# Attention, slot mixture and squared-ReLU layer on one core: a place in SBUF freed early for one slice of mixing weights, half an expert in the tokens' place, expert weights in longer rows, and combine weights transposed elsewhere

## What is computed

```python
# 1. attention: batch 4, heads 8, 768 positions, head size 64
scores = q @ k.T / 8 - slope[h] * dist;  keep: first 8 keys, or 0 <= row - col < 96
x = softmax(scores) @ v                      # as 3072 tokens x 512
# 2. soft mixture: 8 experts with 4 slots each, F = 1024
logits = x @ phi                             # 3072 x 32
d = softmax over the tokens; slot_input = d.T @ x              # 32 x 512
slot_out[e] = relu(slot_input[e] @ w1[e]) @ w2[e]              # w1 512x1024, w2 1024x512
x = softmax over the slots (logits) @ slot_out
# 3. x = relu(x @ w_in) ** 2 @ w_out          # w_in 512x2048, w_out 2048x512
```

## Time and profile before

| | us |
|---|---|
| median of three runs | 513.3 (512.65 to 513.88) |
| the profiled execution, its own time | 512.37 |
| its span, first to last instruction | 510.6 |
| TensorE busy | 485.2 (95%) |
| VectorE busy | 363.6 (71%) |
| ScalarE busy | 346.4 (68%) |
| GpSimd busy | 95.1 (19%) |
| chain that ended last, TensorE's share | 80% |

### The profile page before, as it was taken

One profiled execution on the slowest core, in us unless ns is written; L12 is line 12 of the kernel. 1 busy time (PEld: TensorE's weight loads), 2 busy tenths in 40 slices (PEclk: granted clock), 3 DMA queues, 4 the chain that ended last, 5 costly groups with the idle time before them and its releaser, 6 DMA issues.

```text
span 510.6 us, 12851 instructions
## 1 busy us (share of the span) xinstructions
PE 485.2 (95%) x4608; PEld 399.3 (78%) x4608; DVE 363.6 (71%) x1026; ACT 346.4 (68%) x761; POOL 95.1 (19%) x223
## 2 busy tenths in 40 slices
PE   2999999999999998869989999999999999999997
PEld 1767766776766642325879999999999999999996
DVE  6687786786786662226998978777777877768783
ACT  2788887887888710004999887777677777777740
POOL 1555544554454404120000000000000000000000
PEclk9999999999999999999999999999999999999999
DMA  7699889884465599997001011010110101001011
GB/s 287 245 348 355 348 292 320 328 333 151 151 207 162 202 352 407 391 387 283 0 1 43 1 43 42 0 41 0 41 38 3 41 0 41 5 36 41 0 42 42
DMA packets 24587, 77.24 MB, mean 151 GB/s; under 512 B 2400, under 2 KB 2400, under 8 KB 22112
## 3 DMA queue, kind: packets, MB, share of 16 engines
q1 hardware_dynamic: 19536, 60.95, 32.8%
q10 hardware_dynamic: 5008, 15.73, 8.3%
HBM read 70.39 MB, written 6.29 MB: 150 GB/s over the span
## 4 chain that ended last, share of the span: by engine, by line
PE 80%; ACT 6%; DVE 3%; SPq 3%; DMA 3%; issue 2%; POOL 2%; ACTq 0%; DVEq 0%; POOLq 0%
PE bank L1579 14%; PE bank L1578 14%; PE bank L1580 14%; PE bank L1251 8%; PE bank L1239 5%; PE bank L1266 4%; PE bank L1550 4%; SPq L387 3%; PE bank L1271 3%; ACT probs L990 3%; PE bank L1301 2%; DMA w_b<-w_dram 2%; POOL probs L443 2%; PE bank L1234 2%; PE bank L1509 2%
## 5 line engine op out<-in xcount | busy, mean ns | idle before, releaser
L990 ACT ACTIVATE probs<-probs,nmax 128x232 f32<-128x232 f32 (+1 forms) x192 | 88.6, 462 | 33.6 <-DVE nmax L533 33.6
L443 POOL TENSOR_SCALAR probs<-probs,rden 128x232 f32<-128x232 f32 (+1 forms) x192 | 83.0, 453 | 92.0 <-DVE rden L542 92.0
L1578 PE MATMUL bank<-t_hi,s_hi 128*128 128x256 f32 x352 | 98.7, 280 | 0.0
L1579 PE MATMUL bank<-t_lo,s_hi 128*128 128x256 f32 x352 | 98.6, 280 | 0.0
L1580 PE MATMUL bank<-t_hi,s_lo 128*128 128x256 f32 x352 | 98.5, 280 | 0.0
L533 DVE CUSTOM_DVE_ANT_0 probs<-bank,bias 128x232 f32<-128x232 f32 (+1 forms) x192 | 61.7, 378 | 25.5 <-PE bank L1239 22.1
L1113 ACT ACTIVATE g_s<-bank 128x1024 f32<-128x1024 f32 x48 | 49.0, 1022 | 30.2 <-PE bank L1550 30.2
L1142 ACT ACTIVATE s_hi<-s 128x512 fp32r<-128x512 f32 x88 | 55.0, 627 | 18.5 <-DVE s L917 14.6
L1578 PEld LDWEIGHTS bank<-t_hi,s_hi 128*128 128x128 f32 x352 | 66.5, 189 | 0.0
L1579 PEld LDWEIGHTS bank<-t_lo,s_hi 128*128 128x128 f32 x352 | 66.4, 189 | 0.0
L1580 PEld LDWEIGHTS bank<-t_hi,s_lo 128*128 128x128 f32 x352 | 66.4, 189 | 0.0
(11 more groups left out here) (189 smaller groups left out, 995.3 us busy)
## 6 DMA issues: line engine op xcount, KB each, us to landing
qkv_s<-qkv_dram SPq DMA_DIRECT2D x15, 1028.0 KB, 7.6
qkv_s<-qkv_dram SPq DMA_DIRECT2D x16, 704.0 KB, 4.9
w_s<-w_dram ACTq DMA_DIRECT2D x5, 2048.0 KB, 11.4
w_s<-w_dram SPq DMA_DIRECT2D x15, 512.0 KB, 8.5
out_dram<-o_stage SPq DMA_DIRECT2D x24, 256.0 KB, 2.0
w_a<-w_dram SPq DMA_DIRECT2D x9, 512.0 KB, 10.3
wo_raw<-w_out_dram SPq DMA_DIRECT2D x4, 1024.0 KB, 13.6
w_pre<-w_dram ACTq DMA_DIRECT2D x1, 2048.0 KB, 10.1
```

The source lines that it names most:

```text
L443: last = pool.tensor_scalar(probs[:, v % 2, m, a, 0:w], probs[:, v % 2, m, a, 0:w], rden[:, v % 2, m, a:a + 1], 1.0, ALU.mult, ALU.mult)
L990: act.activation(probs[:, v % 2, m, a, 0:w], probs[:, v % 2, m, a, 0:w], ACT.Exp, bias=nmax[:, v % 2, m, a:a + 1], scale=-1.0, accum_out=d ...
L1578: pe.matmul(OUT[n], hi, W_HI[n](at_f), start=(c == 0 and f == 0 and n in (0, 2, 4, 5)), stop=False, skip_group_check=True)
L1579: pe.matmul(OUT[n], hi, W_LO[n](at_f), start=False, stop=False, skip_group_check=True)
```

## The change

- The bias tables are split in heads 0 to 5 and heads 6 and 7. The first six heads' tables are no longer read when three steps of the last batch are left; the second 1 MB slice of w_in (`win_a[1]`) goes there. SyncE issues it, and `win_c[1]`, ahead of blocks 4 and 5 of expert 2. The other slice, `win_a[0]`, stays where the 2 MB `win_a` was issued.
- The first half of w2 of expert 7 goes into the tokens' place in REG_C (`w2_c`), behind `slots_1`, the last reading of the tokens. The second half (`w2_b`) follows the last chunk of w1.
- w2 is laid out as `e (p c) n`: partition p holds rows 8 p to 8 p + 7, and a load of n blocks has rows of 2n KB. `ht_g` reads `h_s` with a step of 8 elements to match. w_out is laid out in pairs of rows (4 KB), and mix is written in that order, from PSUM with a step of 2 elements.
- `W2_PARTS` are 4, 2, 1 and 1 blocks, of three experts each (6 MB in all).
- `parts(0)` stands behind `l2_0`, `parts(1)` behind `l1_1`, `parts(2)` ahead of block 0 and `parts(3)` ahead of block 4 of `l2_1`. VectorE's `spread` (3 operations) moves from ahead of `relu_0` to behind the copy of `parts(2)`.

```diff
@@ REG_A, REG_B, REG_C
-        bias = at(REG_A, "bias", [P, HEADS, KW])
-        bias0 = at(REG_A, "bias0", [P, HEADS, P])
+        bias_last = at(REG_A, "bias_last", [P, 2, KW])
+        bias0_last = at(REG_A, "bias0_last", [P, 2, P])
+        win_1 = cursor[REG_A]
+        bias0_first = at(REG_A, "bias0_first", [P, HEADS - 2, P])
+        bias_first = at(REG_A, "bias_first", [P, HEADS - 2, KW])
...
+        win_at = win_1 - 8192
-        win_a = at(REG_A, "win_a", [P, DC // 2, FF])
+        win_a = [at(REG_A, "win_a0", [P, FF], start=win_at), at(REG_A, "win_a1", [P, FF])]
-        w2_b = at(REG_B, "w2_b", [P, FEC, D], start=0)
+        w2_b = at(REG_B, "w2_b", [P, FEC // 2, D], start=0)
+        w2_c = at(REG_C, "w2_c", [P, FEC // 2, D], start=8192)
-        W2_PARTS = ((0, 2), (2, 4), (4, 6), (6, 7), (7, 8))
+        W2_PARTS = ((0, 4), (4, 6), (6, 7), (7, 8))
-        w2_v = w2.rearrange("e (c p) n -> e p c n", p=P)
+        w2_v = w2.rearrange("e (p c) n -> e p c n", p=P)
@@ SyncE
             load_w2(2, 0, 4)
+            if windowed:
+                sp.wait_ge(biased, 8 + BATCH * (2 * UNITS) - 4 * GRP)
+                load_win(1)
+                sp.wait_ge(nat_ready, LAST * STEPS + (SLOT_HALF[1] + 1))
+                load_win(3)
             sp.wait_ge(pv_done, 2 + BATCH * UNITS - TILES)
             load_w2(2, 4, 6)
             if windowed:
-                sp.wait_ge(nat_ready, LAST * STEPS + (SLOT_HALF[1] + 1))
-                load_win(3)
                 sp.wait_ge(scores_ready, BATCH * STEPS)
...
-            sp.dma_start(win_a[:, :, :], win_v[:, 0:DC // 2, :]).then_inc(win_in, 16)
+            load_win(0)
+            sp.wait_ge(mid_pe, pe_at["slots_1"])
...
+            sp.dma_start(w2_c[:, :, :], w2_v[7, :, 0:FEC // 2, :]).then_inc(w2_c_in, 16)
...
-            for part in range(2):
-                load_w2_part(part, (3,))
+            sp.dma_start(w2_b[:, :, :], w2_v[7, :, FEC // 2:FEC, :]).then_inc(w2_b_in, 16)
             sp.wait_ge(mid_pe, pe_at["l2_0"])
-            for part in range(len(W2_PARTS)):
-                load_w2_part(part, range(3 if part < 2 else 4))
+            for part, (f0, f1) in enumerate(W2_PARTS):
+                for j in range(3):
+                    sp.dma_start(w2_of(1, j, f0, f1), w2_v[4 + j, :, f0:f1, :]).then_inc(w2_part[part], 16)
...
-                sp.dma_start(wo_raw[:, blocks, :], w_out.rearrange("(c p) n -> p c n", p=P)[:, blocks, :]).then_inc(wo_in[n], 16)
+                sp.dma_start(wo_raw[:, blocks, :].rearrange("p (i r) n -> p i r n", r=2),
+                             w_out.rearrange("(i p r) n -> p i r n", p=P, r=2)[:, 2 * n:2 * n + 2, :, :]).then_inc(wo_in[n], 16)
@@ VectorE and ScalarE, mix
-                dve.tensor_copy(mix[:, n * 512:(n + 1) * 512], bank[4 + n][:, :]).then_inc(mix_dve, 1)
+                dve.tensor_copy(mix_blocks(n), bank[4 + n][:, :].rearrange("p (i q r) -> p i r q", i=2, r=2)).then_inc(mix_dve, 1)
@@ TensorE
+                if g == 1:
+                    parts(1)
                 pe.wait_ge(mid_act, act_at[f"relu_{g}"])
                 dve(f"relu_{g}")
                 for f in range(FEC):
-                    last = pe.transpose(bank[2 + f // 4][:, (f % 4) * P:(f % 4 + 1) * P], h_s[:, f * P:(f + 1) * P], ident[:, :])
+                    last = pe.transpose(bank[2 + f // 4][:, (f % 4) * P:(f % 4 + 1) * P], h_s[:, bass.ds(f, P, step=FEC)], ident[:, :])
...
-                    if g == 1 and f % 2 == 0:
-                        parts(f // 2)
+                    if g == 1 and f in (0, FEC // 2):
+                        parts(3 if f else 2)
...
+                            pe.wait_ge(w2_part[[f0 for f0, _ in W2_PARTS].index(f)], 3 * 16)
+                        if g == 1 and j == 0 and f in (0, FEC // 2):
+                            pe.wait_ge(w2_b_in if f else w2_c_in, 16)
...
                 mark(last, f"l2_{g}")
                 if g == 1:
                     idle_products(3, 3)
+                else:
+                    parts(0)
```

More of the change, by code:

```diff
@@ L281, in build @@
         DVE_M = ["log_t"] * windowed + ["max_row", "disp", "neg_diff", "w_sum", "slot_acc_0", "fold_n", "slot_acc_1", "si_t", "comb_rec",
-                 "relu_0", "h_t_0", "so_0", "so_t_0",
-                 "relu_1", "h_t_1", "comb_t_0", "comb_t_1", "comb_t_2", "comb_t_3", "so_1", "so_t_1", "mix_gl_0", "mix_gl_1"]
+                 "relu_0", "h_t_0", "so_0", "comb_t_0", "so_t_0",
+                 "relu_1", "comb_t_1", "h_t_1", "comb_t_2", "comb_t_3", "so_1", "so_t_1", "mix_gl_0", "mix_gl_1"]
         pe_at = {m: n + 1 for n, m in enumerate(PE_M)}
@@ L298, in w1_of, with w2_of, mix_blocks @@
             return w1_c if (g, j) == (1, 0) else w1_s[j]
-        def w2_of(g, j):
+        def w2_of(g, j, f0, f1):
+            if (g, j) == (1, 3):
+                return w2_c[:, f0:f1, :] if f1 <= FEC // 2 else w2_b[:, f0 - FEC // 2:f1 - FEC // 2, :]
             places = ((w2_s0, w2_pre, w2_a[:, 0:FEC, :], w2_a[:, FEC:2 * FEC, :]),
-                      (w2_s0, w2_a[:, 0:FEC, :], w2_a[:, FEC:2 * FEC, :], w2_b))
-            return places[g][j]
+                      (w2_s0, w2_a[:, 0:FEC, :], w2_a[:, FEC:2 * FEC, :]))
+            return places[g][j][:, f0:f1, :]
+        def mix_blocks(n):
+            return mix[:, n * 512:(n + 1) * 512].rearrange("p (i r q) -> p i r q", i=2, r=2)
         def before(b, s, lag):
@@ L319, in load_win @@
             def load_win(c):
-                sp.dma_start(win_c[c - 2][:, :], win_v[:, c, :]).then_inc(win_in, 16)
+                sp.dma_start((win_a[c] if c < 2 else win_c[c - 2])[:, :], win_v[:, c, :]).then_inc(win_in, 16)
             def load_v(k, n):
@@ L530, in bias_scores @@
                         for a in range(2):
-                            b_ap = bias0[:, 2 * p + a, :] if i0 + m == 0 else bias[:, 2 * p + a, :]
+                            b_ap = bias0_of(2 * p + a) if i0 + m == 0 else bias_of(2 * p + a)
                             dve.tensor_tensor_reduce(
@@ L762, in _ @@
                 if g == 1:
-                    for b in range(BATCH):
-                        pe(f"parts_{b}")
-                        own(dve.tensor_copy(comb_t[:, b * SEQ:b * SEQ + 4 * P], bank[0][:, :]), S2)
-                        mark(dve.tensor_copy(comb_t[:, b * SEQ + 4 * P:(b + 1) * SEQ], bank[1][:, 0:SEQ - 4 * P]), f"comb_t_{b}")
+                    copy_comb(2)
+                    for r, times in ((0, 0.0), (2, 1.0), (4, 0.0)):
+                        own(dve.tensor_scalar(spread[:, :, r:r + 2, :], ident[:, :].rearrange("p (n s) -> p n s", n=4).unsqueeze(2)
+                                              .broadcast_to([P, 4, 2, SLOTS]), times, None, ALU.mult), S2)
+                    copy_comb(3)
                 pe(f"l2_{g}")
                 mark(dve.tensor_copy(h_s[:, 0:D], bank[6][:, :]), f"so_{g}")
+                if g == 0:
+                    copy_comb(0)
                 pe(f"st_{g}")
@@ L1520, in _ @@
             dve("so_t_1")
-            pe.wait_ge(win_in, 48)
+            pe.wait_ge(win_in, 64)
             for h in range(2):
                 for c in range(DC):
-                    win = win_a[:, c, :] if c < DC // 2 else win_c[c - DC // 2]
+                    win = win_a[c] if c < DC // 2 else win_c[c - DC // 2]
                     for n in range(4):
```

43 lines of the change are left out of this document (23 added, 20 removed).

## The result

| us | before | change |
|---|---|---|
| median | 512.97 (512.46 to 513.88, 4 runs) | 508.56 (508.01 to 510.36, 4 runs) |
| profiled execution, own time | 512.37 | 510.36 |
| its span | 510.6 | 508.6 |
| last block of `l2_1` starts | 230.54 | 228.55 |

The ratio is 0.9926, with a 95% interval of 0.9906 to 0.9946: faster, by 2.8 to 4.8 us. So the trace shows the slowest of these four. Not all of that mean stands for lost time: at the very end of the kernel (504 to 508 us) the granted clock is 0.84, as in the tail of the kernel before, and what follows the last block of `l2_1` takes the same time in both. Lines L... are now those of the changed kernel.

A forecast was written before the change was run, and what follows sets the result against it. It took `l2_1` as bound by bytes of w2; moved bytes and longer rows put its last block at 227.3 us instead of 230.54, 3.3 us earlier, so 513.3 - 3.3 = 510.0 us, range 508.9 to 511.9.

The forecast's parts named there:

- What bounds the kernel, and that the end follows the stage: `l2_1` is bound by bytes of w2 (5.1 us of TensorE stops); its earlier end reaches the kernel's end in full.
- Part 0 whole at 218.9: In `l2_1`, w2's first part, 3 MB in 8 KB rows, takes 7.35 us from 211.5 and lands at 218.9 us.
- TensorE decides, last block at 227.3: End of `l2_1`: 8.4 us of TensorE work from 218.9 ends after the last part's 226.8; the stage gains 3.3 us.
- the sum's last line: Whole kernel: the 3.3 us gain taken from the runs' median, 513.3 us, giving 510.0 us.
- Rows: Loads of w2: 2.45 us a MB in 8 KB rows, 2.71 in 2 KB; gain 3.3 us, without faster rows 2.2.
- rows don't matter: Rival on the w2 loads: only bytes count, so the gain is 2.2 us, 511.1 us; chance 0.15.
- Bytes: DMA queue: 1 MB of `win_a` moves early at no cost, leaving 6 MB of w2 behind `l2_0` instead of 7.
- Gaps buy nothing: `parts(0)` and `parts(1)`, 0.87 us each, moved into TensorE's idle gaps gain nothing, as TensorE waited for DMA anyway.
- Stepped reading: Transposes of `h_s` and copies of mix from PSUM, both read with a step: no cost taken for either.
- Mix copies: Rival after `l2_1`: stepped copies of mix are slow, so the gain is 2.2 us, 511.1 us; chance 0.12.
- my second bound: ScalarE's two stepped copies of mix twice as long, 1.09 us more on the path; the gain would be 2.2 us.
- TensorE resumes at half speed: Rival in `l2_1` after a 3.3 us idle: brief 511 to 513 us (0.07), long 514.1 or 519.4 us (0.04).

The follow-up runs named there:

- the second measure: The steady kernel with w_out in rows of 2 KB and mix written in its old order: 507.77 us, ratio 0.9907.
- the steady kernel: The change plus twelve unread products in the pause ahead of block 0 of `l2_1`, without idle products before the last block: 508.00 us, ratio 0.9907.

## Why the prediction was right, and where it was off

Faster, with a chance of 0.88, and 508.56 us against 510.0 us, just below the range's low end of 508.9 as a time, while the ratio times 513.3 us is 509.5. That a later six runs of the change have a median of 510.46 us, nearer to 510.0, is luck: it comes from the dip, which the sum doesn't hold. Step by step:

- **What bounds the kernel, and that the end follows the stage: right.** The rest behind the last block is 281.8 us in all fourteen profiles.
- **Part 0 whole at 218.9: right.** 218.68 (change) and 218.41 us or earlier (pause filled). The last part, forecast for 226.8, is there at 226.17 (226.68 in the second measure).
- **TensorE decides, last block at 227.3: right in kind, 0.45 us too late.** Undisturbed it is 226.85: part 0 is 0.2 us sooner, and the sum of 8.4 us for blocks, `parts(3)` and `idle_products` measured 8.17.
- **The step that failed is the sum's last line**, 513.3 - 3.3. I had 512.37 - 3.3 = 509.1 us against the profiled execution, and 226.85 + 281.8 = 508.65 us is what the undisturbed change takes by its trace. The 0.9 us that I put on top, because the median of before lay above its profiled execution, did not carry over: that surplus belongs to executions of before whose clock dips (median 513.09 against 511.88 us, above), or to chance, and is no constant of the kernel. With the 0.45 us above it makes the 1.4 us.
- **Rows: right in kind, and rather too small.** I had 1.1 us for the stage (3.3 - 2.2), 1.2 us at the last transfer (228.0 - 226.8). Measured there are 1.87 and 1.36 us, against two executions with long rows, and 1.24 us at the first block on the first chip. One thing was missed: `w2_c` itself has long rows too, another 0.26 us for its megabyte. What is left, up to 0.4 us, stays open. The stretch from 190 to 195 us doesn't explain it: seven profiles with long rows and all the moves have 331 to 357 GB/s there, the two with rows of 2 KB 347 and 311. In the kernel before, the last parts moved at 387 GB/s; in the steady kernel parts 2 and 3, still in rows of 2 KB, moved at 397 GB/s (222 to 226 us) beside w_out's longer rows. The rival "rows don't matter" is out: from 205 to 215 us the two kernels with rows of 2 KB move 387 to 396 GB/s, all with 8 KB rows there 419 to 428.
- **Bytes: right in kind.** I gave each moved megabyte its full 2.6 to 2.7 us. The half expert comes near that (2.2 us, worked out above from the kernel without it); the late slice of w_in costs less, 1.15 us in one comparison and 0.6 to 1.9 us over all of them, since it fills room that stays empty otherwise.
- **Gaps buy nothing: borne out by the trace for the kernel before, wrong for the change.** With loads as before the blocks start when DMA says (the 0.9 us of the medians stays open). In the change TensorE decides, and both `parts` taken out of their gaps and put in the pause cost 0.6 us. I had worked out that TensorE decides "just", and didn't go back to this sentence with it.
- **Stepped reading.** Transposes of `h_s`: 1.13 us instead of 1.06, a cost of 0.07 us, hidden. Mix copies: nothing, the rival is out. The Trainium skill's note on cachelines (SBUF — State Buffer) would have had both pay for each new line, and gives no size; the doubled copies of my second bound were my own reading of it. For the PSUM copies no run here shows a cost, for the transposes the trace shows 7%.
- **TensorE resumes at half speed: the rival that was priced too low.** I gave it 0.11, long or brief. A clock below full comes in 1 of 4 and 5 of 6 executions of the change; the two that were profiled have it in the brief form behind the pause, and it costs 1.7 and 2.6 us; "511 to 513 us" was the place (509.8 to 511.6 measured), and the sign stays. My reason against it, "60 us of steady work", was wrong: in both profiles the dip stands right behind the pause (3.51 and 3.26 us), and filling it with idle products, with nothing else changed, leaves six of six runs at a full clock (on another chip, on which other kernels dip too). The Trainium skill (TensorE: Matmul & The Clock Gate, HAM oscillation) says that a wait for DMA between bursts puts the engine back to 1.2 GHz. Here that holds for some executions of one kernel and not for others.

**The best version seen** is the change with the pause filled and no idle products ahead of the last block: 508.0 us. With w_out in rows of 2 KB it is 507.8 us, the same ratio. Its lead over the change, on other chips, is up to 0.7 us where the change's clock is full (508.0 to 508.7 us) and 1.8 to 3.6 us where it dips.

## What to carry to other kernels

A load that is merged to save waits makes one long stop out of several short ones; read how long TensorE stands then, and keep it turning or cut the stop in two, because a dip of the clock behind it can eat half of the gain in some executions and none in others. When a change takes a stage from one bound to another, go through everything "hidden" under the old bound again: in the traces, work in a gap bought nothing while DMA decided and 0.6 us when TensorE did. And add a forecast's difference to the execution that it was read from; a surplus of the median over it is noise or a state of its own, not a constant to carry over.

## What the runs showed of the hardware

- **The dip is a matter of the execution.** With the same kernel and nearly the same pause (3.51 and 3.26 us) the slow stretch began at the fourth row or at the first and lasted 3.4 or 5.1 us; executions with a full mean clock exist beside them (508.09 us at 1.000 on the chip where the other five were below it). With pauses of 4.52 and 4.59 us in the profile (late slice, rows of 2 KB) none of 14 runs was at 0.999 or more. A stop of 2.51 us did it in the kernel before with moved `parts`, where 2.69 us didn't in the profile of before; with stops of 1.35 and 1.53 us one run of six has a clock of 0.997. Where a run that was not profiled loses its clock is not shown; the mean alone says that it does.
- **Idle products hold the clock.** With twelve of them in the pause and 0.56 to 0.68 us of it left (three kernels, 17 runs) the mean clock was 0.999 or 1.000 each time. With 2.33 us left (rows of 2 KB) and 1.78 us left (late slice) one of six runs each was at 0.995.
- **Row length sets the rate of a standing queue**: 386 to 389 GB/s at 2 KB, 406 to 411 at 4 KB (200 to 205 us), 419 to 428 at 8 KB (205 to 215 us). The Trainium skill (DMA: Bandwidth & Descriptors, Where 436 GB/s comes from) has the HBM side bind a load at about 358 GB/s, though it calls a measured 425 GB/s for 16 MB near the other, higher limit; all three rates here are above the first, and the longest rows reach the second.
